# A three-stage fp32 kernel on one core: state-output products on all 128 rows, a copy moved to ScalarE, and a new order of the attention steps

## What is computed

```python
# attention: batch 4, heads 8, sequence 768, head dim 48
for t in range(S):
    cur = u * k[t] (outer) v[t]
    y[t] = r[t] @ (state + cur)
    state = w[t][:, None] * state + k[t] (outer) v[t]
# ffn: x (3072 x 384), w1, w2 (384 x 1024), w3 (1024 x 1024), w_out (1024 x 384)
h = (x @ w1) * (x @ w2) @ w3
x2 = h @ w_out
# top-2 mixture of 8 experts: noisy gates from x2, per expert relu(x2 @ ew1[e]) @ ew2[e]
```

## Time and profile before

| | us |
|---|---|
| median of three runs | 998.77 (998.05 to 1001.21) |
| the profiled execution | 999.43 |
| its span, first to last instruction | 997.7 |
| PE busy in the span | 955.2 (96%) |
| DVE busy | 689.9 (69%) |
| ACT busy | 523.7 (52%) |

### The profile page before, as it was taken

The page is one execution under the profiler, slowest core; times in us unless marked ns, Lnnn a source line. Parts: engine busy times, 40 slices in busy tenths (PEclk is TensorE's granted clock), DMA queues, the critical chain, the costliest instruction groups (busy, mean ns, idle before and its releaser), DMA issues.

```text
span 997.7 us, 18088 instructions
## 1 busy us (share of the span) xinstructions
PE 955.2 (96%) x6825; PEld 902.0 (90%) x6825; DVE 689.9 (69%) x1161; ACT 523.7 (52%) x970; POOL 222.0 (22%) x209
## 2 busy tenths in 40 slices
PE   4999999999999999999999999999999999999995
PEld 3655999989998999999999999999999999999995
DVE  7889777879696978263778585765857658576570
ACT  2545444355453545234545575665756657566560
POOL 0000000110202020203344323333332432323311
PEclk8999999999999999999999999999999999999998
DMA  8986433352425220306348797877978779787751
GB/s 255 285 262 204 128 112 107 107 171 85 132 83 173 69 70 29 102 1 229 111 167 265 198 296 213 243 257 209 302 208 245 257 211 299 208 246 254 215 154 16
DMA packets 87307, 179.02 MB, mean 179 GB/s; under 512 B 18914, under 2 KB 44260, under 8 KB 87220
## 3 DMA queue, kind: packets, MB, share of 16 engines
q1 hardware_dynamic: 73844, 157.18, 49.5%
q0 software_dynamic: 12976, 20.66, 9.9%
q10 hardware_dynamic: 400, 0.02, 0.0%
HBM read 152.22 MB, written 26.97 MB: 180 GB/s over the span
## 4 chain that ended last, share of the span: by engine, by line
PE 80%; DVE 12%; issue 3%; ACT 2%; DMA 1%; SPq 0%; POOL 0%; DVEq 0%; ACTq 0%; POOLq 0%
PE bank L1209 20%; PE pp L1225 20%; PE bank L780 10%; PE bank L797 6%; PE fx L780 4%; PE yu L1268 3%; PE fx L797 3%; DVE kdiv L258 2%; PE pp L186 2%; PE tr L1190 2%; PE yu L1250 1%; PE fx L1250 1%; DVE work L865 1%; PE yu L230 1%; PE yu L207 1%
## 5 line engine op out<-in xcount | busy, mean ns | idle before, releaser
L1118 POOL DMA_INDIRECT result<-x2s,who x55 | 92.9, 1689 | 286.8 <-ACT x2s L1342 273.9
L1329 DVE SCALAR_TENSOR_TENSOR abl<-bank,abh 128x512 fp32r<-128x512 f32 x96 | 66.2, 690 | 109.9 <-ACT abh L1324 109.9
L969 POOL DMA_INDIRECT slot_entry<-entry,slot_i x48 | 50.3, 1048 | 352.9 <-DVE token_f L958 340.7
L1209 PE MATMUL bank<-xh,set_up_h 128*128 128x256 f32 x384 | 109.2, 284 | 0.0
L1209 PE MATMUL bank<-xh,set_up_l 128*128 128x256 f32 x384 | 108.6, 283 | 0.0
L1209 PE MATMUL bank<-xl,set_up_h 128*128 128x256 f32 x384 | 108.6, 283 | 0.0
L1324 ACT ACTIVATE abh<-bank 128x512 fp32r<-128x512 f32 x96 | 57.5, 599 | 81.3 <-PE bank L1209 81.2
L780 PE MATMUL bank<-xh,w12h 128*128 128x384 f32 x264 | 89.7, 340 | 1.4 <-DVE xl L477 0.9
L780 PE MATMUL bank<-xh,w12l 128*128 128x384 f32 x264 | 88.4, 335 | 0.0
L780 PE MATMUL bank<-xl,w12h 128*128 128x384 f32 x264 | 88.2, 334 | 0.0
L1225 PE MATMUL pp<-set_down_h,abh 128*128 128x384 f32 x256 | 87.7, 342 | 0.0
(11 more groups left out here) (260 smaller groups left out, 2650.5 us busy)
## 6 DMA issues: line engine op xcount, KB each, us to landing
up_raw<-in_moe_w SPq DMA_DIRECT2D x93, 512.0 KB, 4.6
down_raw<-in_moe_w SPq DMA_DIRECT2D x124, 384.0 KB, 4.8
vs<-in_v_rows SPq DMA_DIRECT2D x16, 384.0 KB, 3.4
wt<-in_w SPq DMA_DIRECT2D x32, 144.0 KB, 2.8
kt<-in_k SPq DMA_DIRECT2D x32, 144.0 KB, 2.8
rt<-in_r SPq DMA_DIRECT2D x32, 144.0 KB, 3.0
kn<-in_k_rows SPq DMA_DIRECT2D x16, 288.0 KB, 3.3
rn<-in_r_rows SPq DMA_DIRECT2D x16, 288.0 KB, 4.8
```

Source lines behind the costliest of these rows:

```text
L969: nc.gpsimd.indirect_dma_start(slot_entry, bass.IndirectOffsetOnAxis(slot_i[:, s, n:n + 1], 0), entry[:, s, n, :], None).then_inc(scattere ...
L1118: nc.gpsimd.indirect_dma_start(out, bass.IndirectOffsetOnAxis(who[v % 4][:, s, 0:1], 0), yo[v % 2][:, s, 0:DM], None, bounds_check=N - 1, ...
L1209: last = nc.tensor.matmul(bank[m % 2][:, f * T2:(f + 1) * T2], wp[:, kk, c:c + P], xp[:, kk, :], start=(n == 0), stop=(n == 3 * KD - 1))
L1329: nc.vector.scalar_tensor_tensor(hl[:, 2 * m:2 * m + 2, :].rearrange("p a t -> p (a t)"), bank[m % 2][:, :], 0.0, hh[:, 2 * m:2 * m + 2, : ...
```

## The change

The states' output products (L225, now L224) take all 128 rows: `state` becomes [P, 5, 2, 64], with head 0's state in rows 0 to 63 of plane 0 and zeros in its other rows, and the reverse in plane 1, and the padding rows of `rt` (so of `rdec`) are filled with 0 in place of 1. ACT therefore writes each state in two halves, ten instructions a pair in place of five. DVE's copy out of `yu` becomes ACT's (`act_products`). `added` and `ruk` have one buffer in place of two. In the slots, derive 2 stands with "out", derive 3 one slot and derive 4 and 5 one and two slots earlier, and the parts of `diag` stand in other slots (the last behind derive 4). The first three `w3_mm` steps stand ahead of the first scores. The "turn" of a next batch stands one part of "down" later. SP clears behind the second store and doesn't wait for the token load.

```diff
-        ruk = [asb(f"ruk{i}", [P, NC, 2, D]) for i in range(2)]
+        ruk = asb("ruk", [P, NC, 2, D])
-        added = [asb(f"added{i}", [P, NC - 1, D]) for i in range(2)]
-        state = [asb(f"state{i}", [P, NC - 1, HB]) for i in range(2)]
+        added = asb("added", [P, NC - 1, D])
+        state = [asb(f"state{i}", [P, NC - 1, 2, HB]) for i in range(2)]
...
-                        rows = slice(h * HB, h * HB + D)
                         nc.tensor.matmul(output_bank(c // 3)[h * HB:(h + 1) * HB, c % 3 * C:(c % 3 + 1) * C],
-                                         state[q % 2][rows, c - 1, :], rdec[q % 2][rows, c * C:(c + 1) * C],
+                                         state[q % 2][:, c - 1, h, :], rdec[q % 2][:, c * C:(c + 1) * C],
                                          start=c in (1, 3), stop=False, skip_group_check=True)
...
+        def act_products(act, b, q):
+            g = HP * b + q
+            act.wait_ge(yu_full, 3 * g + 1)
+            nc.scalar.copy(added[:, :, :], yu[:, 0:(NC - 1) * D].rearrange("p (c x) -> p c x", c=NC - 1)
+                           ).then_inc(yu_free, 1)
...
-                nc.scalar.activation(state[q % 2][:, c, 0:D], added[q % 2][:, c, :], ACT.Copy,
-                                     scale=decay[q % 2][:, c, C:C + 1]).then_inc(state_ready, 1)
+                for h in range(2):
+                    rows = slice(h * HB, (h + 1) * HB)
+                    nc.scalar.activation(state[q % 2][rows, c, h, 0:D], added[rows, c, :], ACT.Copy,
+                                         scale=decay[q % 2][rows, c, C:C + 1]).then_inc(state_ready, 1)
...
-                     [("out", q, 0), ("out", q, 1)],
-                     [("derive", q + 1, 2)],
-                     [("derive", q + 1, 3)], [("derive", q + 1, 4)], [("derive", q + 1, 5)], []]
-            for part, at in enumerate((3, 4, 5) if first else (0, 4, 5)):
+                     [("out", q, 0), ("out", q, 1), ("derive", q + 1, 2)],
+                     [("derive", q + 1, 3)],
+                     [("derive", q + 1, 4)], [("derive", q + 1, 5)], [], []]
+            for part, at in enumerate((3, 5, 6) if first else (0, 5, 6)):
...
+            front, build = front + build[:3], build[3:]
...
-                    for x in (wt, kt, rt):
-                        nc.vector.memset(x[i][HB // 2:HB, :], 1.0)
-                        nc.vector.memset(x[i][HB + HB // 2:2 * HB, :], 1.0).then_inc(turned_clear, 1)
+                    for x, pad in ((wt, 1.0), (kt, 1.0), (rt, 0.0)):
+                        nc.vector.memset(x[i][HB // 2:HB, :], pad)
+                        nc.vector.memset(x[i][HB + HB // 2:2 * HB, :], pad).then_inc(turned_clear, 1)
...
-            TURN_AT = 4
+            TURN_AT = 5
...
-                            if n == 0:
+                            if (q, n) == (HP - 1, 0):
+                                sp_group_load(sp, b + 1, 0)
+                            if n == 1:
                                 sp_clear(sp, HP * b + q)
                                 sp.wait_ge(zeros_stored, 16 * (HP * b + q + 1))
-                            if (q, n) == (HP - 1, 0):
-                                sp_group_load(sp, b + 1, 0)
-                                sp.wait_ge(xr_loaded[0], 16 * (b + 2))
```

More of the change, by code:

```diff
@@ L220, in pe_output @@
                 pe.wait_ge(att_ready, 2 * g + 2)
-                pe.wait_ge(state_ready, (NC - 1) * (g + 1))
+                pe.wait_ge(state_ready, 2 * (NC - 1) * (g + 1))
                 for c in range(1, NC):
                     for h in range(2):
-                        rows = slice(h * HB, h * HB + D)
                         nc.tensor.matmul(output_bank(c // 3)[h * HB:(h + 1) * HB, c % 3 * C:(c % 3 + 1) * C],
-                                         state[q % 2][rows, c - 1, :], rdec[q % 2][rows, c * C:(c + 1) * C],
+                                         state[q % 2][:, c - 1, h, :], rdec[q % 2][:, c * C:(c + 1) * C],
                                          start=c in (1, 3), stop=False, skip_group_check=True)
@@ L244, in dve_decays @@
             dve.wait_ge(loaded[0][q % 2], 32 * (2 * b + q // 2 + 1))
-            need(dve, state_ready, (NC - 1) * (g - 1))
+            need(dve, state_ready, 2 * (NC - 1) * (g - 1))
             for c in range(NC):
@@ L280, in dve_products @@
                     dve.wait_ge(rows_loaded[n][i], 16 * (2 * b + q // 2 + 1))
-                need(dve, diag_ready, g - 1)
-                nc.vector.tensor_tensor(ruk[i][:, :, :, :], kn[i][:, :, :, :], rn[i][:, :, :, :], ALU.mult).then_inc(rk_ready, 1)
+                need(dve, diag_ready, g)
+                nc.vector.tensor_tensor(ruk[:, :, :, :], kn[i][:, :, :, :], rn[i][:, :, :, :], ALU.mult).then_inc(rk_ready, 1)
             else:
@@ L287, in dve_products @@
                 one = u_all[:, q, :, :].rearrange("p h d -> p (h d)")
-                nc.vector.tensor_tensor(ruk[q % 2][:, :, :, :].rearrange("p c h d -> p c (h d)"),
-                                        ruk[q % 2][:, :, :, :].rearrange("p c h d -> p c (h d)"),
+                nc.vector.tensor_tensor(ruk[:, :, :, :].rearrange("p c h d -> p c (h d)"),
+                                        ruk[:, :, :, :].rearrange("p c h d -> p c (h d)"),
                                         bass.AP(one.tensor, one.offset, [one.ap[0], [0, NC], [1, 2 * D]]),
@@ L297, in dve_diag @@
             nc.vector.reduce_sum(diag[:, :, :].rearrange("p c h -> p (c h)"),
-                                 ruk[q % 2][:, :, :, :].rearrange("p c h d -> p (c h) d"), axis=AX.X).then_inc(diag_ready, 1)
+                                 ruk[:, :, :, :].rearrange("p c h d -> p (c h) d"), axis=AX.X).then_inc(diag_ready, 1)
         causal_bits = causal[:, :].bitcast(i32)
@@ L326, in dve_state @@
             g = HP * b + q
[L327 to L330, removed]
             dve.wait_ge(yu_free, g + 1)
@@ L333, in dve_state @@
                 need(dve, state_step, (NC - 2) * g + c - 1)
-                nc.vector.scalar_tensor_tensor(added[q % 2][:, c, :], added[q % 2][:, c - 1, :], decay[q % 2][:, c - 1, C:C + 1],
-                                               added[q % 2][:, c, :], ALU.mult, ALU.add).then_inc(state_step, 1)
+                nc.vector.scalar_tensor_tensor(added[:, c, :], added[:, c - 1, :], decay[q % 2][:, c - 1, C:C + 1],
+                                               added[:, c, :], ALU.mult, ALU.add).then_inc(state_step, 1)
+        def act_products(act, b, q):
[3 more added lines that the diff above has]
+                           ).then_inc(yu_free, 1)
         def act_state(act, b, q):
@@ L410, in act_attention @@
             b, q = later(b, q)
-            if step == "scale":
+            if step == "state":
+                act_products(act, b, q)
+            elif step == "scale":
                 act_state(act, b, q)
@@ L590, in first_pool @@
                 for i in range(2):
-                    nc.gpsimd.memset(state[i][:, :, D:HB], 0.0).then_inc(pad_zero, 1)
+                    nc.gpsimd.memset(state[i][:, :, :, :], 0.0).then_inc(pad_zero, 1)
                 nc.gpsimd.memset(gates[:, :, 2 * E:4 * E], 0.0).then_inc(gates_clear, 1)
```

## The result

The changed kernel takes 1011.56 us (median of four runs, 1009.25 to 1012.58) where the kernel before, beside it, takes 999.69: a ratio of 1.0096, 95% interval 1.0070 to 1.0121. It is slower by about 1%, 12 us, where 998.7 and a range of 993 to 1004 were forecast. The profiled execution took 1009.25 us with a span of 1007.5, 9.8 more than before's 997.7.

A forecast was written before the change was run, and what follows sets the result against it. PE bounds the second phase, a chain mostly through DVE the first. From 999.43 us, 8.7 gained in the second phase and 8.1 lost in the first give 998.8, taken as 998.7; 8-in-10 range 993 to 1004.

The forecast's parts named there:

- Ten state writes: ACT's state writes, ten for five: about 2.4 us, 0.2 late in six pairs, 1.1 us lost (0 to 2).
- Waits for `att`: Second phase: DVE reaches the mask 1.06 us sooner, so PE's five 0.8 us waits go; 4.0 us gained (0 to 4.0).
- The batch's end: Second phase: earlier token load, `kdiv` and `rdec` not behind the token split; PE's waits go, 4.0 us gained.
- What is next late there: Second phase, after the `att` waits go: PE itself was named as next late.
- State products on all rows: PE's output: no 0.15 us tile-form crossing per pair; 1.8 us gained in the second phase, 0.3 in the first.
- (d): Rival: full-height weight loads don't hide, 20 bare loads in each of 16 pairs, 42.6 us, 1041 us; chance 0.03.
- The start: First phase: weight steps ahead delay first scores to 26.3 and decays to 32.8; 3.1 us lost (1.2 to 3.8).
- The middle: First phase: `w12l` ahead of `rdec` and ACT's later `att` writes; 2.2 us lost (0 to 4.5), clock taken as 0.
- The end: First phase: `diag` ends later, behind the last reciprocal and `kdiv`; 2.1 us lost (1.8 to 2.3).
- The clock: PE pauses about 3.5 us before the first "up" product, second phase may begin at half rate; 1.0 us lost (0 to 2).
- (b): Rival: the start decides for slower, half clock behind weight products and every later pause; 12.3 us lost, 1003.0 us; chance 0.18.
- (a): Rival: clock stays up in the first phase, only 4.0 us lost there (start 1.2), 994.7 us; chance 0.31.

The follow-up runs named there:

- the halves in turn: Changed kernel with its ten state writes reordered: five to rows 0 to 63, then five to rows 64 to 127; 1003.3 us, ratio 1.0009.
- the first phase as before: Changed kernel, state writes half by half, no weight steps ahead, first-phase slots of the kernel before, new order kept in the second phase; 996.9 us, ratio 0.9932.
- The same kernel with quarters: The 996.9 us kernel with state products back on 48-row quarters and five state writes; 996.4 us, ratio 0.9929.
- the places alone: Kernel before with only the second phase's new places, later "turn", new queue order, and one buffer each for `added` and `ruk`; 1001.2 us, ratio 0.9944.
- the run with two waits on PE: The 996.9 us kernel with PE waiting for and multiplying head 0's five states, then head 1's; 1002.1 us, ratio 0.9996.

## Why the prediction was wrong, by its steps

**Ten state writes: the step that failed.** The sum had ten at the pace of five, 2.4 us, 0.2 us late in six pairs, 1.1 lost. They took 3.55, late by 1.40 in six pairs and about 0.24 in five: 9.6 us. The assumption marked in the text was right as far as it went (a 64-row write is as long as a 128-row one, 333 and 326 ns); that two neighbours on different halves don't overlap was not in the bound of 0 to 2, though five in 1.23 us, each of 0.33, show that overlap is there to be lost. The other six pairs, taken to have 1 us to spare or more, were late too in five cases. The order of the writes is worth 8.3 us in the changed kernel (1011.6 to 1003.3), 7.0 of them in the second phase. With the rest as before it is about 16 by the ratios (1.0142 to 0.9983), with 7 on either side; between the two traces it is 9.9 in the span and 8.9 in the second phase.

**Waits for `att`: right.** 4.0 us in 5 before, none after. **The batch's end: right** in that its waits are gone, 3.9 us; the 0.2 counted at a third boundary was the wait at 98.38, which is in the first phase. **What is next late there: wrong.** PE itself was named; it was ACT's `work`, 0.5 us in each of five groups, 2.3 us.

**State products on all rows: right.** The rows above show L229's second group 0.65 us behind its first, no crossing, and the rival (d) without ground. This is the weight loads and matmuls of one pair, in the changed kernel (minimum, median and longest ns, first and last start):

```profile
L224 PEld LDWEIGHTS pp<-rdec,state x12: 137/137/137, 117.4 to 118.0; 128*64 128x64 f32 x12
L224 PE MATMUL pp<-rdec,state x12: 272/272/273, 117.5 to 118.1; 128*64 128x128 f32 x12
```

Twelve records start within 0.6 us, 0.055 each, with loads of 0.137 that use all rows, as the matmuls in flight do. The rule of the Trainium skill, TensorE: Matmul & The Clock Gate, Part 3 (Packing small matmuls), that a load overlaps only with matmuls of another row group, would have made the kernel 1041 by the estimate of (d); the trace doesn't agree with it here.

**The second phase's sum.** With the halves in turn and the first phase as before it is 309.3 us, a gain of 3.7. By the steps: 1.8 + 4.0 + 3.9, less 2.0 for states and 2.3 for `work`, is 5.4. With alternation, 1.8 + 7.9 less 9.6 and 2.3 is -2.2, and -4.8 was measured. PE's busy time in the phase has most of these 1.7 and 2.6 us: 304.9 and 305.7 for 305.2 before, where the crossings should have made it 303.4. The same kernel with quarters has 306.2 (and the places alone 306.0), so the crossings did save 1.3, and 1.0 came with the new order. How the new order adds to PE's busy time is not settled.

**The first phase, forecast 8.1, measured 4.9.** The start was right: first scores at 25.98 (26.3), first decays at 32.56 (32.8).

```profile
20.31 5.74 PE L673 MATMUL fx<-wo,w3T 128*128 128x400 f32 x12 [2.88 <-DVE wo L622]
25.98 0.94 PE L186 MATMUL pp<-rdec,kdiv 48*128 48x128 f32 x12
```

The middle was forecast at 2.2 and measured at 0.1 (fourth decays 89.02 for 86.08, of which 2.8 are the start's): the cold scores at 59.48 went, as counted (none of this phase's before 84 us takes over 0.94), and only part of the rest was lost. The pauses counted at 3.2 and 2.0 us ahead of the second and third pairs' scores were 1.57 (at 44.45) and none. The end was right, 1.9 for 2.1 (89.02 to 105.79 for 86.08 to 100.92). The clock was forecast to fall at the start of the second phase, 1.0 us; it fell before that, in 80 to 101, behind waits of 1.59 and 0.22 us. The changed kernel's PE there:

```profile
84.23 1.24 PE L186 MATMUL pp<-rdec,kdiv 48*128 48x128 f32 x12 [1.59 <-DVE att L319]
85.70 1.31 PE L207 MATMUL yu<-vs,kend_t 128*64 128x48 f32 x20 [0.22 <-issue]
86.94 5.22 PE L673 MATMUL fx<-wo,w3T 128*128 128x400 f32 x8
```

That is about 3.1 us more on PE than at full clock. The chain that ended last runs through all three rows, but a second one ends with it. PE's last weight products, which ACT casts next, end at 102.99, and ACT's twelve `att` writes behind the fourth `diag` at 102.93 (a row of the chain, then one of ACT in order of time):

```profile
97.60 5.39 PE bank L673 x16
```
```profile
99.31 3.62 ACT L311 ACTIVATE att<-ident,diag 128x128 f32<-128x128 f32 x12 [1.18 <-DVE diag L296]
```

So of the 3.1 us the 2.3 of the weight products cost less than 0.1, since ACT was busy as long. The 0.8 of the scores and of L207 stand also ahead of the fourth decays, since DVE's steps wait for ACT's copy of L207's products: they are on both chains. The middle's 0.1 holds them, and without the clock it would be 0.7 gained. The clock cost 0.8 where 1.0 was forecast, at another place, and none at the start of the second phase.

What could not be priced from the profile is how the two edits of this phase act together. Undone singly they give 0.1% (on the changed kernel as it is) and 0.3% (on the one with halves in turn), each within the intervals, and together 0.8% (1.0009 to 0.9932, with halves in turn). Each delays the chain between DVE and PE, and either alone is enough for some of PE's pauses; that this is the mechanism is argued, not shown.

**The rivals.** None of them was it. (b) had the right sign by a slow first phase, which lost 4.9 us and not 12. The first phase alone came out nearest to (a), 105.79 for its 105, but by other terms: (a) had the start at 1.2, where it was 2.8. No rival had the writes, though their pace stood among the assumptions. Priced afterwards as a rival, with no overlap at all, by the 0.33 us of one write before and the 0.03 between two in the changed kernel: ten are 3.6, from 159.12 to 162.7, 1.4 us behind PE's loads at 161.34 in six pairs; the other six start at least 1 us sooner, 0.4 late; 10.8 us in all, and 999.43 - 9.8 + 10.8 + 8.1 = 1008.5. That this comes near the profiled 1009.25 is in part luck: it has 8.1 for the first phase, which lost 4.9, and 1.0 for the second, which lost 4.8.

## What to carry over

On ACT, instructions that are to be split over halves of the rows should be ordered so that neighbours stay on one half: here that order alone was worth 0.9% of the changed kernel, and 1.6% (0.7 on either side) on the kernel before. Price an added instruction not by its duration nor by the pace of others, but by start to start of the very form and neighbour that it will have, and where the trace has no such row, take the full duration as the far bound. On TensorE it was the reverse: products half as wide as the array lost 6.0 us when neighbours stayed on one column half. The gain of this change lay in the places of a few steps in the second phase, which alone give 0.6% (which of them was not tested singly), and not in the products.

## What the hardware showed

- ACT: five or ten `activation` writes of 48 elements start every 0.23 to 0.24 us if neighbours are on the same rows (128x48, or 64x48 in turn: 2.37 and 2.49 us for ten), and every 0.36 if they go between rows 0 to 63 and 64 to 127 (3.55 us). The median duration of one is 323 to 333 ns in each case.
- PE: 128\*64 records with 137 ns loads start 0.055 us apart with the column halves in turn, and 0.11 apart within one half (the run with two waits on PE).
- The granted clock fell to 0.50 behind waits of 1.59 and 0.22 us (changed kernel, 84 us), and of 1.79 (with weight steps ahead, 82 us), and held at 1.00 behind others of like length (1.51 at 87 us without the steps ahead, 1.40 in the second phase) and behind a longer one, 2.77 us at 55.20 in the changed kernel:

```profile
55.20 0.66 PE L224 MATMUL yu<-rdec,state 128*64 128x128 f32 x8 [2.77 <-ACT state L349]
```

  The granted clock of the changed kernel is 1.00 in the stretch from 55 to 58 us and 0.50 from 85 to 87. No rule is drawn from these cases.
